# Moved routing steps, input transposes in larger groups and a reordered last batch in an attention and mixture-of-experts kernel

## The reference

```python
scores = scale * q @ k.T + bias            # 8 heads of 64, causal, window 128
x = softmax(scores) @ v                    # 2304 x 512

logits = x @ w_gate                        # 8 experts, each takes at most 288 tokens
for idx in argsort(-logits.flatten()):     # greedy, over all (token, expert) pairs
    tok, e = idx // E, idx % E
    if assigned[tok] < 0 and counts[e] < 288:
        assigned[tok] = e; counts[e] += 1
y[assigned == e] = relu(x[assigned == e] @ w1[e]) @ w2[e]     # 512 -> 1024 -> 512

h = y @ w_in                               # 512 -> 2048
out = (h * sigmoid(h)) @ w_out             # 2048 -> 512
```

## Time and profile before

| | |
|---|---|
| median of 3 runs | 928.77 us (927.79 to 928.84) |
| the profiled execution | 928.7 us |
| its span, first to last instruction | 927.0 us |
| mean granted TensorE clock | 0.971 |
| TensorE matmul, 0 to 185 us (attention) | 178.29 us busy |
| TensorE matmul, 185 to 236 us (first routing) | 18.05 us busy, granted clock 0.53 |
| GpSimd, share of the span | 32% |
| DMA, mean over the span | 77 GB/s |

### The profile page before, as it was taken

One profiled execution on the slowest core, in us unless ns is written; L12 is line 12 of the kernel. 1 busy time (PEld: TensorE's weight loads), 2 busy tenths in 40 slices (PEclk: granted clock), 3 DMA queues, 4 the chain that ended last, 5 costly groups with the idle time before them and its releaser, 6 DMA issues.

```text
span 927.0 us, 17883 instructions
## 1 busy us (share of the span) xinstructions
PE 857.6 (93%) x6792; PEld 796.7 (86%) x6792; DVE 496.3 (54%) x1685; ACT 345.6 (37%) x814; POOL 298.6 (32%) x298
## 2 busy tenths in 40 slices
PE   7999999932999999999999999999999999999996
PEld 6999999931988898889889888988898889899995
DVE  6666666556657457455745561656457455732110
ACT  5666656502324333423432242324333432433221
POOL 1422222414125223522522262326123522523222
PEclk9999999955999999999999999999999999999998
DMA  6666666303303213030312120303212030321000
GB/s 159 154 149 149 154 155 151 105 14 117 92 1 118 67 49 92 26 112 4 117 55 60 53 65 1 125 3 116 68 48 92 27 115 1 117 69 46 1 1 34
DMA packets 117253, 71.43 MB, mean 77 GB/s; under 512 B 61616, under 2 KB 103600, under 8 KB 117168
## 3 DMA queue, kind: packets, MB, share of 16 engines
q1 hardware_dynamic: 114192, 60.85, 24.0%
q0 software_dynamic: 2976, 9.44, 3.3%
HBM read 60.83 MB, written 9.44 MB: 76 GB/s over the span
## 4 chain that ended last, share of the span: by engine, by line
PE 65%; DVE 10%; ACT 1%; issue 1%; DMA 1%; POOL 1%; SPq 0%; DVEq 0%; POOLq 0%
PE hp L1033 11%; PE hp L1035 10%; PE hp L1034 10%; PE acc L1092 6%; PE acc L1094 6%; PE acc L1093 6%; PE acc L1033 4%; PE acc L1034 4%; PE acc L1035 4%; PE rt L977 3%; DVE test L1214 1%; DVE h_raw L1438 1%; ACT gate L1172 1%; DVE closing L1281 1%; DMA rows<-x_rows,tokens 1%
## 5 line engine op out<-in xcount | busy, mean ns | idle before, releaser
L960 POOL TENSOR_TENSOR h_l<-h_raw,h_h 128x256 fp32r<-128x256 f32 (+1 forms) x128 | 107.8, 842 | 266.5 <-ACT h_h L1180 266.3
L1033 PE MATMUL hp<-xy_h,res_h 128*128 128x256 f32 (+1 forms) x512 | 155.1, 303 | 0.8
L1034 PE MATMUL hp<-xy_l,res_h 128*128 128x256 f32 (+1 forms) x512 | 151.7, 296 | 0.0
L1035 PE MATMUL hp<-xy_h,res_l 128*128 128x256 f32 (+1 forms) x512 | 151.7, 296 | 0.0
L1438 DVE TENSOR_TENSOR h_raw<-hp,gate 128x256 f32<-128x256 f32 (+1 forms) x128 | 58.2, 455 | 173.8 <-ACT gate L1172 173.8
L946 POOL TENSOR_TENSOR wb_l<-wb_raw,wb_h 128x512 fp32r<-128x512 f32 x64 | 87.5, 1369 | 177.3 <-ACT wb_h L1126 175.8
L1172 ACT ACTIVATE gate<-hp 128x256 f32<-128x256 f32 (+1 forms) x128 | 52.3, 409 | 178.2 <-PE hp L1035 175.1
L1092 PE MATMUL acc<-res_h,h_h 128*128 128x512 f32 x288 | 116.9, 406 | 0.0
L1093 PE MATMUL acc<-res_l,h_h 128*128 128x512 f32 x288 | 113.5, 394 | 0.0
L1094 PE MATMUL acc<-res_h,h_l 128*128 128x512 f32 x288 | 113.5, 394 | 0.0
L1033 PEld LDWEIGHTS hp<-xy_h,res_h 128*128 128x128 f32 x512 | 97.3, 190 | 6.0 <-issue 2.3
(11 more groups left out here) (212 smaller groups left out, 1800.3 us busy)
## 6 DMA issues: line engine op xcount, KB each, us to landing
wa_raw<-in_moe_w_dram SPq DMA_DIRECT2D x64, 256.0 KB, 4.1
wb_raw<-in_moe_w_dram SPq DMA_DIRECT2D x64, 256.0 KB, 3.1
q_rows<-in_q_dram SPq DMA_DIRECT2D x32, 128.0 KB, 3.5
k_rows<-in_k_dram SPq DMA_DIRECT2D x32, 128.0 KB, 2.7
v_rows<-in_v_dram SPq DMA_DIRECT2D x32, 128.0 KB, 2.4
stage<-in_moe_w_in_dram SPq DMA_DIRECT2D x8, 512.0 KB, 4.6
x_rows<-x_rows_sb SPq DMA_DIRECT2D x16, 256.0 KB, 4.2
stage<-in_moe_w_out_dram SPq DMA_DIRECT2D x8, 512.0 KB, 4.6
```

Of the source, the lines that this page charges most:

```text
L960: pool.tensor_tensor(h_l[:, cols], h_raw[:, cols], h_h[:, cols].bitcast(FP32), ALU.subtract).then_inc(g_low, 1)
L1033: nc.tensor.matmul(out_, weights_h, cols_h, start=start, stop=False)
L1034: nc.tensor.matmul(out_, weights_h, cols_l, start=False, stop=False)
L1035: return nc.tensor.matmul(out_, weights_l, cols_h, start=False, stop=stop)
```

## The change

The diff does five things.

- `setup()` of the next expert moves from slot +0 to slot +3.
- The 17 hooks move to +7, +8, +10, +11, +13, +14, +16, +17, +19, +20, +22, +23, +25, +29, +33, +35, +37. With them move the loads of the next expert's first tiles (by hook 12, two slots), the fetch (by hook 14, four slots), and the splitting of the first four tiles (by hook 12 + 6, two slots: +31, +33, +35, +37).
- The inputs are turned in four banks at once ahead of b13; chunk 0 uses the `hp` bank that a0 of the next stage will use, chunk 3 uses `acc[2]`. Where the running batch is 384 rows wide (`acc[2]` is in use then), three chunks are turned ahead of b13 and the fourth ahead of b15.
- In the last dense stage b14 and b15 are merged: for each row tile first the three matmuls of b14, then those of b15.
- SyncE, not GpSimd, waits at the end for the last scatters.

```diff
--- before.py
+++ after.py
@@ -672,8 +672,8 @@
 ROUNDS = 2 * len(STEPS)
 HOOKS = 2 * ROUNDS + 5
 
-SETUP_AT = {FIRST[2 * _j - 2]: _j for _j in range(1, E)}
-HOOK_LIST = {_j: [FIRST[2 * _j - 2] + _n for _n in (5, 6, 8, 9, 11, 12, 14, 15, 17, 18, 20, 21, 23, 25, 29, 30, 32)]
+SETUP_AT = {FIRST[2 * _j - 2] + 3: _j for _j in range(1, E)}
+HOOK_LIST = {_j: [FIRST[2 * _j - 2] + _n for _n in (7, 8, 10, 11, 13, 14, 16, 17, 19, 20, 22, 23, 25, 29, 33, 35, 37)]
              for _j in range(1, E)}
 HOOK_AT = {_n: (_j, _h) for _j, _list in HOOK_LIST.items() for _h, _n in enumerate(_list)}
 HOOK_AT[0] = (0, HOOKS - 1)
@@ -692,8 +692,10 @@
 
 X_AT = {}
 for _j in range(1, E):
-    X_AT[AT[2 * _j - 1, "b", FT2 - 3]] = [(_j, 0), (_j, 1)]
-    X_AT[AT[2 * _j - 1, "b", FT2 - 2]] = [(_j, 2), (_j, 3)]
+    _late = BATCH[_j - 1][1] > 2 * P
+    X_AT[AT[2 * _j - 1, "b", FT2 - 3]] = [(_j, _c) for _c in range(DC - _late)]
+    if _late:
+        X_AT[AT[2 * _j - 1, "b", FT2 - 1]] = [(_j, DC - 1)]
 
 RING = 4
 
@@ -716,7 +718,7 @@
 for _w in range(RING, E * FT1):
     _s, _f = tile_stage(_w)
     if _f < RING:
-        _n = max(FIRST[_s - 1] + 13, HOOK_LIST[_w // FT1][2 * ROUNDS] + 4) + 2 * _f
+        _n = max(FIRST[_s - 1] + 13, HOOK_LIST[_w // FT1][2 * ROUNDS] + 6) + 2 * _f
         SPLIT_A.setdefault(_n, []).append(_w)
         SPLIT_B.setdefault(_n, []).append(_w)
     else:
@@ -867,7 +869,11 @@
 
             if j == 0:
                 return acc[c]
-            return tp if c % 2 == 0 else acc[DC - 1]
+            if c == 0:
+                return hp[(A_NO[2 * j, 0] - 1) % 2]
+            if c == 2:
+                return acc[DC - 1]
+            return tp if c == 1 or BATCH[j - 1][1] > 2 * P else acc[2]
 
         @block.sync
         def _(sp):
@@ -890,6 +896,7 @@
                     sp.dma_start(wb_raw[w % RING][:],
                                  w2[bass.ds(e, 1), P * f:P * (f + 1), :].rearrange("o p m -> (o p) m")
                                  ).then_inc(wb_loaded[w % RING], 16)
+            sp.wait_ge(scattered, 16 * TILES_OUT[-1])
 
         @block.gpsimd
         def _(pool):
@@ -964,7 +971,6 @@
                 if n in FETCH_AT:
                     fetch(FETCH_AT[n])
             store(len(BATCH) - 1)
-            pool.wait_ge(scattered, 16 * TILES_OUT[-1])
 
         @block.tensor
         def _(pe):
@@ -1007,19 +1013,6 @@
                                                 start=(t == 0), stop=(t == NT - 1))
                 last.then_inc(pe_part, 1)
 
-            def turn_x(j, c, bank):
-
-                if c == 0:
-                    pe.wait_ge(gathered, (j + 1) * (16 * GR))
-                if j >= 1 and c == 1:
-                    pe.wait_ge(y_low, j * DC)
-                elif j >= 1 and c >= 2:
-                    pe.wait_ge(x_low, j * DC + c - 1)
-                for a in range(GR):
-                    last = nc.tensor.transpose(bank[:, GT * a:GT * (a + 1)], rows[:, a, P * c:P * (c + 1)],
-                                               ident[0:GT, 0:GT])
-                last.then_inc(xt_done, 1)
-
             def bank_free(no):
 
                 s, f = A_SLOTS[no - 1]
@@ -1027,6 +1020,20 @@
                     pe.wait_ge(relu_low, FT1 * STAGES[s][1] + f + 1)
                 else:
                     pe.wait_ge(g_done, FT2 * STAGES[s][1] + f + 1)
+
+            def turn_x(j, c, bank):
+
+                if c == 0:
+                    pe.wait_ge(gathered, (j + 1) * (16 * GR))
+                    if j >= 1:
+                        bank_free(A_NO[2 * j, 0] - 2)
+                        pe.wait_ge(y_low, j * DC)
+                if j >= 1 and c == 3 and bank is tp:
+                    pe.wait_ge(x_low, j * DC + 2)
+                for a in range(GR):
+                    last = nc.tensor.transpose(bank[:, GT * a:GT * (a + 1)], rows[:, a, P * c:P * (c + 1)],
+                                               ident[0:GT, 0:GT])
+                last.then_inc(xt_done, 1)
 
             def product(out_, weights_h, weights_l, cols_h, cols_l, start, stop):
 
@@ -1083,18 +1090,30 @@
             def dense_b(s, k, f):
 
                 tiles = BATCH[k][1] // P
-                pe.wait_ge(g_low, FT2 * k + f + 1)
+                fs = [f]
+                if s == len(STAGES) - 1 and f >= FT2 - 2:
+
+                    if f == FT2 - 2:
+                        return
+                    fs = [FT2 - 2, FT2 - 1]
+                    pe.wait_ge(g_low, FT2 * k + FT2 - 1)
+                else:
+                    pe.wait_ge(g_low, FT2 * k + f + 1)
                 if f == 0:
                     pe.wait_ge(y_low, (STAGES[s - 1][1] + 1) * DC)
-                o = FT2 * DM + DM * f
                 for t in range(tiles):
-                    m = slice(COLS * (f % 3) + P * t, COLS * (f % 3) + P * (t + 1))
-                    nc.tensor.matmul(acc[t][:], h_h[:, m], res_h[:, o:o + DM], start=(f == 0), stop=False)
-                    nc.tensor.matmul(acc[t][:], h_h[:, m], res_l[:, o:o + DM], start=False, stop=False)
-                    last = nc.tensor.matmul(acc[t][:], h_l[:, m], res_h[:, o:o + DM], start=False, stop=(f == FT2 - 1))
+                    for b in fs:
+                        o = FT2 * DM + DM * b
+                        m = slice(COLS * (b % 3) + P * t, COLS * (b % 3) + P * (t + 1))
+                        if t == 0 and b > fs[0]:
+                            pe.wait_ge(g_low, FT2 * k + FT2)
+                        nc.tensor.matmul(acc[t][:], h_h[:, m], res_h[:, o:o + DM], start=(b == 0), stop=False)
+                        nc.tensor.matmul(acc[t][:], h_h[:, m], res_l[:, o:o + DM], start=False, stop=False)
+                        last = nc.tensor.matmul(acc[t][:], h_l[:, m], res_h[:, o:o + DM], start=False,
+                                                stop=(b == FT2 - 1))
                     if f == FT2 - 1 and t < tiles - 1:
                         last.then_inc(acc_done, 1)
-                last.then_inc(b_done, 1)
+                last.then_inc(b_done, len(fs))
 
             for h in range(HOOKS - 1):
                 if h == 1:
```

## The result

The changed kernel takes 904.16 us, the median of 4 runs (903.57 to 905.37); before, 4 runs on the same chip give 928.68 (927.79 to 928.84). The ratio is 0.974, 95% interval 0.9723 to 0.9756: 2.6% faster. Forecast were 900.1 us and a range of 897.8 to 907.5. The profiled execution took 903.57 us, its span is 901.8.

A forecast was written before the change was run, and what follows sets the result against it. The prediction took TensorE to bound the kernel, its matmuls busy for 93% of the span, with time to gain only where it stands still or at the end. Its terms summed to -28.6 us: 928.7 to 900.1 us, range 897.8 to 907.5.

The forecast's parts named there:

- setup to +3: Expert stages, a2's start: with setup no longer ahead of a0's `h_l`, seven waits go, -10.6 us.
- hook 13: Dense stage: four slots instead of two behind hook 12 remove seven waits for `row_pair`, -8.2 us.
- hook 15: Dense stage: a slot between hook 14 and hook 15 removes six waits, -2.6 us.
- turning the inputs: Ahead of b13: one turn instead of two saves 0.7 us, six times, -4.2 us; the 384-row case saves 0.
- into the dense stage: Expert to dense stage: hook 6's products cover the chain that made a0 start late seven times, -2.0 us.
- what is late next: Dense stage, b10 and a14: GpSimd's backlog behind the fetch costs 0.3 us, six times, +1.8 us.
- the end: Last dense stage: last scatter over earlier, -1.0 us; GpSimd's drain starts at the last issue's end, -1.8 us.
- Rival 2: Dense stage: GpSimd's backlog makes b10 or a14 wait 1.2 to 1.5 us in six 256-row batches; 907 us, chance 0.17.
- Rival 3: Expert stages: setup's stall moves to hook 1 or a5, VectorE late by 1 us in seven stages; 907.5 us, chance 0.06.
- Rival 1: The end: GpSimd's drain counts from the landing of the scatters, 1.8 us more; 901.9 us, chance 0.2.
- Rival 4: Turn of the rows at +45: the gather comes late, slower than before with a landing over 13.5 us; 930 us, chance 0.01.
- Rival 5: Whole kernel: the edits do not act because other waits hold each slot; within 2 us of 928, chance 0.02.

The follow-up runs named there:

- experiment 1: The changed kernel with setup() put back from slot +3 to slot +0: 916.18 us.
- experiment 8: Three kernels, each undoing one part of the changed kernel: inputs turned in pairs, 908.56 us; GpSimd waits for the landing, 906.63; b14 and b15 apart, 906.42.
- experiment 10: The kernel of experiment 9 with hook 13 back at +27, two slots behind hook 12: 905.92 us.
- experiment 3: The changed kernel with GpSimd's and VectorE's low parts of each expert's first four tiles two slots later: 902.18 us.
- experiment 6: The changed kernel with hook 13 back at +27, two slots behind hook 12, and hook 14 left at +33: 904.79 us.
- experiment 2: The changed kernel with only GpSimd's low parts of each expert's first four tiles two slots later: 901.14 us.
- experiment 7: The changed kernel with hooks 13 and 14 at +28 and +32, one slot earlier each, and the fetch with hook 14: 905.66 us.
- experiment 5: The changed kernel with hooks 15 and 16 two slots later (+37, +39) and the fetch at +39: 905.49 us.
- experiment 4: The changed kernel with hooks 15 and 16 two slots later (+37, +39): 933.69 us.
- experiment 9: The changed kernel with the first four tiles' high parts one slot later and low parts two: 897.46 us, ratio 0.9656 to the kernel before.

## Why the prediction was right, and where it wasn't

The time is 4.1 us above the forecast and inside the range. The steps, with what the runs showed in place of each (us; experiments 1, 8 and 10 without the first stage's clock):

| step | forecast | shown | by |
|---|---|---|---|
| setup to +3 | -10.6 | -10.6 | experiment 1 |
| hook 13 | -8.2 | -8.3 | experiment 10 |
| hook 15 | -2.6 | +5.6 | 6 x (1.36 - 0.43), both timelines |
| turning the inputs | -4.2 | -3.8 | experiment 8 |
| into the dense stage | -2.0 | -2.0 | 7 x (0.42 - 0.13), both timelines |
| what is late next | +1.8 | 0 | list of waits |
| the end | -2.8 | -3.0 | both spans; experiment 8 has +1.9 and +1.1 |

The column adds up to -22.1. With 1.2 us ahead of the first expert product and 0.6 of the first stage's clock it is 23.9 of the 25.15 by which the spans differ. Of the other 1.3, about 0.5 is the seventh wait for `h_l`, which experiment 1 didn't bring back; the rest isn't assigned. The into-the-dense-stage step was not undone by itself.

Four of the seven terms are right in size and mechanism (setup, hook 13, into the dense stage, the end), and the turning nearly. That the total is off by only 4.1 us is in part luck: hook 15 alone is 8.2 us off, and what made up for it is the stall that didn't come (1.8), the parts that no edit touched (1.8) and the unassigned rest. The upper end of the range stood for rivals 2 and 3, not for this stall.

**The step that failed** is hook 15: "`low_a` of the next tile and a9's `h_raw` now stand ahead of `after` of hook 14, but a slot of 1.4 is enough by about 0.3". The right neighbours were named, their costs were not. First, `h_raw` isn't just 0.42 us of VectorE's time: it waits for `gate`, and on ScalarE `gate` stands behind two high parts, so that the slot gained (1.4) went entirely into a later start (1.42). Experiment 3 showed that `low_a` had no part in it. The high parts themselves run late because `after` of hook 13 keeps a8's `h_raw` back (778.02, its `gate` was ready at 775.96): hooks 13 and 14 moved by four slots and the splitting by two, and experiment 6, with hook 13 two slots earlier, has no stall at hook 15. Second, the operations of `after` run beside GpSimd's `low_b`, and the hold adds 0.98 (experiment 2). The prediction applied the hold only to hook 16, where the row of before showed it, and not to the place to which the change brought it.

**What is late next** was worked out right in mechanism and came out at zero because of that same stall: each batch stood still for 1.36 us at hook 15, four slots ahead of b10, and GpSimd had that much more time. In the changed kernel that `h_l` ends at 788.20 and b10 starts at 788.97, 0.77 of slack behind a stall of 1.36; without the stall b10 would start 0.6 us late by this (an estimate). In experiment 7, without the stall, b10 waits 0.75 and the gap is 0.9 us longer than normal, where the forecast took 0.3 from ends of 0 and 1.5. The two terms weren't independent, and the sum treated them as if they were. (The changed kernel's own order without the stall wasn't run; experiment 7 is the nearest to it.) a14 never waited. **Rival 2** as a case, 907 us, didn't come, but its mechanism did in experiment 7.

The rule that the prediction quoted, Trainium skill, "SBUF — State Buffer", section Who interferes with whom, agrees with `liked`, `free` and `wa_l` (two SBUF inputs) held in the presence of GpSimd's operations, and with `h_raw` (one input in PSUM), which kept its 0.42 us beside them (0.42 to 0.43 each time in the changed kernel). Its same section has that `tensor_scalar` too can contend, in a two-port mode; `full<-left`, with one SBUF input, is such an operation and was held for 4.51 us. The prediction used only the half of the rule on two inputs. As to length, the section lets an exclusion last for the whole instruction; the run shows a hold across four in a row, and the row of before, which the prediction called in agreement, already had one across two.

**Rival 1** (the drain counts from the landing) is refuted: the drain ended 3.49 after the last issue in the changed kernel, 1.8 after the landing, and experiment 8 gives back 1.9. **Rival 3** is refuted: neither setup nor hook 0 releases TensorE anywhere. The slack that was counted was enough. **Rival 4**: the gather never came late in the changed kernel; with the fetch six slots later still (experiment 5) it delayed the turn by 0.2 to 0.4 us in six batches. **Rival 5** is out, all edits act. A way to be slower than before was found only outside the rivals: the kernel of experiment 4, with a delay of two slots in hook 15.

## What to carry to other kernels

When a step is moved in a hand-written order, its new neighbours on *every* engine count: here the decisive one was a copy on ScalarE that stood ahead of the input of the neighbour on VectorE. Stalls within the same period can replace each other: five placements (the changed kernel and experiments 5, 6, 7 and 10) all ended within 904 to 906 us, with a stall of 0.9 to 1.4 us per batch at hook 13, hook 15, hook 16 or b10. Only the one that keeps hook 13's distance and also takes away the causes of hook 15's stall (high parts ahead of `gate`, low parts beside `after`) gained the next 7 us. So judge an edit also in the version without the other stall, before calling it worthless. And compare slot by slot where it can be done: differences of 0.5 to 1.1 us in the middle came from when the clock rose, not from the edits.

## What was not expected of the hardware

- **A small VectorE operation can be held for a whole run of GpSimd's.** 128 x 8 elements took 4.51 us (0.3 elsewhere) in experiment 4, 128 x 2 took 4.33 in the changed kernel, `wa_l` 4.82 and 5.10 in experiments 2 and 9 (0.69 otherwise). All four began while GpSimd was issuing the last indirect DMA of the fetch and ended within 0.1 of the end of the fourth operation behind it, `wa_l` 0.56 behind it. But the start beside an issue isn't what it takes: in experiment 3 `wa_l` began at 788.24, while GpSimd computed a `wb_l`, and was held for 4.81 us, across that one and the next four operations (the last ends at 792.49, `wa_l` at 793.05). In experiment 7 an `out_tokens` that began beside an `h_l` was held across the next operation too (1.83 us). `liked` and `free` in the changed kernel also began while GpSimd computed, and were held by one operation only. What decides between the two is open.
- **A standstill of 4.35 us brought the granted clock from 1.00 to 0.50**, for 3.4 us in three batches of experiment 4 and for 6.8 in the other three; those of 1.2 us did not (1.00 throughout the middle of the changed kernel from 232.8 us on). In experiment 4 six waits of 25.8 us in all made the middle 30 us longer, though hook 15's 8 us were saved.
- **GpSimd's drain behind indirect DMAs takes 3.49 us, counted from the end of the last issue or, if a wait puts it later, from its own start**, whether the data has landed or not: it ends at 901.59 with the last issue over at 898.10 in the changed kernel, at 904.45 with 900.96 where b14 and b15 are apart, and it lasts 3.49 from 901.14, behind the landing, in experiment 8. A wait for the landing on another engine is free beside it; on GpSimd it costs its 1.9 us.
